# V tiles by head, filled by one transfer and two halo copies, with q and k loaded further ahead in a fused attention and two-layer feed-forward kernel

## The reference, cut to what matters

```python
def _attn_ref(q, k, v):                     # block 32, window 16
    k_sum = k.reshape(B, H, nb, block, D).max(axis=3)
    v_sum = v.reshape(B, H, nb, block, D).mean(axis=3)
    scores_l = scale * q @ k.T, kept where |i - j| < window
    scores_s = scale * q @ k_sum.T + log(block)
    a = softmax(concat(scores_l, scores_s))
    return a @ concat(v, v_sum)

x = attention, heads side by side           # (1536, 512)
h = x @ w_in;  solu = h * softmax(h);  x = layernorm(solu) * g_ln @ w_out
h = x @ w2_in; out = elu(h) @ w2_out
```

## Time and profile before

| | us |
|---|---|
| median of 3 runs | 538.21 |
| lowest and highest | 536.62, 539.1 |
| the profiled execution | 538.56 |
| its span, first to last instruction | 536.8 |

### The profile page before, as it was taken

One profiled execution on the slowest core, in us unless ns is written; L12 is line 12 of the kernel. 1 busy time (PEld: TensorE's weight loads), 2 busy tenths in 40 slices (PEclk: granted clock), 3 DMA queues, 4 the chain that ended last, 5 costly groups with the idle time before them and its releaser, 6 DMA issues.

```text
span 536.8 us, 8565 instructions
## 1 busy us (share of the span) xinstructions
PE 502.4 (94%) x3312; PEld 420.5 (78%) x3312; DVE 235.5 (44%) x625; ACT 212.6 (40%) x433; POOL 112.3 (21%) x100
## 2 busy tenths in 40 slices
PE   3698879897999999999999999999999999999997
PEld 2476657675779889899988888888888888888885
DVE  2445644652684255455256454423233333333231
ACT  2346634751574346345455443324121223222222
POOL 2263838440012002002445353200000000000000
PEclk9999965999899999999999999999999999999999
DMA  9579596934000000017000000002000002000002
GB/s 176 115 137 229 130 216 147 227 118 206 0 0 2 1 0 1 1 45 269 1 1 0 1 0 2 0 1 78 1 0 0 1 0 78 0 0 0 0 0 78
DMA packets 46402, 30.35 MB, mean 57 GB/s; under 512 B 40096, under 2 KB 40096, under 8 KB 45472
## 3 DMA queue, kind: packets, MB, share of 16 engines
q1 hardware_dynamic: 46368, 29.89, 21.6%
HBM read 25.17 MB, written 3.15 MB: 53 GB/s over the span
## 4 chain that ended last, share of the span: by engine, by line
PE 80%; DMA 5%; SPq 4%; POOL 4%; DVE 3%; ACT 2%; issue 2%; DVEq 0%; POOLq 0%
PE bank L854 12%; PE bank L856 12%; PE bank L855 12%; PE bank L1056 8%; PE bank L1057 8%; PE bank L1055 8%; PE bank L1011 4%; PE bank L1013 4%; PE bank L1012 4%; DMA vblocks<-in_v 3%; PE bank L931 2%; POOL vblocks L406 2%; SPq L311 2%; PE bank L997 2%; PE bank L898 1%
## 5 line engine op out<-in xcount | busy, mean ns | idle before, releaser
L615 ACT ACTIVATE ex<-bank 128x512 f32<-128x512 f32 x48 | 28.7, 598 | 127.9 <-PE bank L856 127.9
L856 PE MATMUL bank<-yt_lo,w2in_hi 128*128 (+1 forms) x192 | 74.7, 389 | 0.0
L855 PE MATMUL bank<-yt_hi,w2in_lo 128*128 (+1 forms) x192 | 74.7, 389 | 0.0
L1055 PE MATMUL bank<-w2out_hi,g_hi 128*128 128x512 f32 x192 | 74.7, 389 | 0.0
L1056 PE MATMUL bank<-w2out_lo,g_hi 128*128 128x512 f32 x192 | 74.7, 389 | 0.0
L854 PE MATMUL bank<-yt_hi,w2in_hi 128*128 (+1 forms) x192 | 74.7, 389 | 0.0
L1057 PE MATMUL bank<-w2out_hi,g_lo 128*128 128x512 f32 x192 | 74.7, 389 | 0.0
L832 DVE TENSOR_SCALAR ex<-ex 128x512 f32<-128x512 f32 x48 | 21.6, 450 | 116.5 <-ACT ex L615 116.5
L837 DVE TENSOR_TENSOR g_lo<-gf,g_hi 128x512 fp32r<-128x512 f32 x48 | 46.5, 969 | 35.9 <-ACT g_hi L623 35.9
L623 ACT ACTIVATE g_hi<-gf 128x512 fp32r<-128x512 f32 x48 | 30.3, 632 | 49.0 <-DVE gf L834 49.0
L498 ACT ACTIVATE se<-se,nm 128x120 f32<-128x120 f32 x96 | 32.5, 387 | 36.4 <-DVE nm L683 36.4
(11 more groups left out here) (103 smaller groups left out, 845.1 us busy)
## 6 DMA issues: line engine op xcount, KB each, us to landing
w2in_raw<-in_w_in SPq DMA_DIRECT2D x1, 4096.0 KB, 12.3
w2out_raw<-in_w_out SPq DMA_DIRECT2D x4, 1024.0 KB, 9.4
kraw<-in_k SPq DMA_DIRECT2D x16, 192.0 KB, 5.3
qraw<-in_q SPq DMA_DIRECT2D x16, 192.0 KB, 4.0
vblocks<-in_v SPq DMA_DIRECT2D x4, 768.0 KB, 8.8
out<-osb SPq DMA_DIRECT2D x12, 256.0 KB, 2.1
vw<-in_v SPq DMA_DIRECT2D x16, 176.0 KB, 6.1
win_raw<-in_w_in SPq DMA_DIRECT2D x4, 512.0 KB, 6.1
```

Of the source, the lines that this page charges most:

```text
L855: pe.matmul(acc, al, bh, start=False, stop=False)
L856: last = pe.matmul(acc, ah, bl, start=False, stop=(i == n - 1))
L1055: pe.matmul(dst, g_hi[:, j % GS, cols], w2out_hi[:, j, :], start=(j == 0), stop=False)
```

## The change

Three things change together.

- vw has its heads outside its windows. One transfer brings both heads' 768 rows to partitions 16 to 79 (64 partitions, 12 windows of each head). Two copies inside SBUF fill the halos: partitions 64 to 79 of each window go to partitions 0 to 15 of the next, and partitions 16 to 31 go to partitions 80 to 95 of the one before. The zeros, the means copy and the matmuls follow the layout.
- Raw k and q have four slots each instead of two.
- SP's list is another one. vblocks(0) stands ahead of q(0), fill_halo(0) ahead of move_means(0), and v(1), vblocks(1), k(2), q(2) are issued ahead of the loop. In round n it is: fill_halo(n + 1), v(n + 2), move_means(n/2 + 1) and vblocks(n/2 + 2) if n is even, k(n + 3), q(n + 3), then w_in or w_out.

```diff
-        (kt, qraw), a1 = place(W2IN, ("kt", [P, 2, HALO + S + HALO], F32), ("qraw", [P, 2, T, P], F32))
+        RAWS = 4
+        (kt, kraw, qraw), a1 = place(
+            W2IN, ("kt", [P, 2, HALO + S + HALO], F32), ("kraw", [P, RAWS, T, P], F32),
+            ("qraw", [P, RAWS, T, P], F32))
...
-            LN, ("kraw", [P, 2, T, P], F32), ("vw", [P, VS, SUBS, 2, D1], F32),
+            LN, ("vw", [P, VS, 2, SUBS, D1], F32),
...
             def load_k(n):
-                if n >= 2:
-                    sp.wait_ge(kv_in_psum, n - 1)
+                if n >= RAWS:
+                    sp.wait_ge(kv_in_psum, n - RAWS + 1)
...
                 else:
                     sp.wait_ge(attn_done, T * (n - VS + 1))
-                for h in range(2):
-                    body = vf[2 * n + h, HALO:HALO + (SUBS - 1) * SUB, :].rearrange("(j i) d -> i j d", i=SUB)
-                    sp.dma_start(vw[2 * HALO:LOCAL, s, 0:SUBS - 1, h, 0:D], body).then_inc(v_loaded[s], 16)
-                sp.dma_start(vw[HALO:2 * HALO, s, 0, :, 0:D],
-                             vf[2 * n:2 * n + 2, 0:HALO, :].rearrange("h i d -> i h d")).then_inc(v_loaded[s], 16)
-                sp.dma_start(vw[2 * HALO:2 * HALO + REST, s, SUBS - 1, :, 0:D],
-                             vf[2 * n:2 * n + 2, S - REST:S, :].rearrange("h i d -> i h d")).then_inc(v_loaded[s], 16)
+                sp.dma_start(vw[HALO:HALO + SUB, s, :, :, 0:D].rearrange("i h j d -> i (h j) d"),
+                             vf[2 * n:2 * n + 2].rearrange("h (j i) d -> i (h j) d", i=SUB)).then_inc(v_loaded[s], 16)
 
             def fill_halo(n):
 
                 s = n % VS
-                sp.wait_ge(v_loaded[s], 16 * V_DMAS * (n // VS + 1))
-                sp.dma_start(vw[0:2 * HALO, s, 1:SUBS, :, :],
-                             vw[SUB:LOCAL, s, 0:SUBS - 1, :, :]).then_inc(halo_filled[s], 16)
+                if n == 0:
+                    sp.wait_ge(zeros_ready, 2)
+                sp.wait_ge(v_loaded[s], 16 * (n // VS + 1))
+                sp.dma_start(vw[0:HALO, s, :, 1:SUBS, :], vw[SUB:SUB + HALO, s, :, 0:SUBS - 1, :]).then_inc(halo_filled[s], 16)
+                sp.dma_start(vw[SUB + HALO:LOCAL, s, :, 0:SUBS - 1, :], vw[HALO:2 * HALO, s, :, 1:SUBS, :]).then_inc(halo_filled[s], 16)
...
             load_k(0)
+            load_vblocks(0)
             load_q(0)
-            load_vblocks(0)
             load_v(0)
             load_k(1)
+            fill_halo(0)
             move_means(0)
-            fill_halo(0)
             load_q(1)
+            load_v(1)
+            load_vblocks(1)
+            load_k(2)
+            load_q(2)
             for n in range(PAIRS):
+                if n + 1 < PAIRS:
+                    fill_halo(n + 1)
+                if n + 2 < PAIRS:
+                    load_v(n + 2)
                 if n % 2 == 0 and n // 2 + 1 < MEANS:
-                    load_vblocks(n // 2 + 1)
-                if n + 1 < PAIRS:
-                    load_v(n + 1)
-                if n + 2 < PAIRS:
-                    load_k(n + 2)
-                    load_q(n + 2)
+                    move_means(n // 2 + 1)
+                if n % 2 == 0 and n // 2 + 2 < MEANS:
+                    load_vblocks(n // 2 + 2)
+                if n + 3 < PAIRS:
+                    load_k(n + 3)
+                    load_q(n + 3)
...
-                if n + 1 < PAIRS:
-                    fill_halo(n + 1)
-                if n % 2 == 0 and n // 2 + 1 < MEANS:
-                    move_means(n // 2 + 1)
...
-            dve.memset(vw[:, :, 0, :, 0:D], 0.0)
-            dve.memset(vw[:, :, SUBS - 1, :, 0:D], 0.0).then_inc(zeros_ready, 1)
+            dve.memset(vw[0:HALO, :, :, 0, 0:D], 0.0)
+            dve.memset(vw[SUB:P, :, :, SUBS - 1, 0:D], 0.0).then_inc(zeros_ready, 1)
```

More of the change, by code:

```diff
@@ L126, in fused_layers_kernel @@
         (vblocks,), _ = place(3 * KD * F1 * 4, ("vblocks", [NB * HPM, 2, BLOCK * D], F32))
-        (kraw, vw, qt, se, pt, vmean, ks, mt, mask, bands, xn), a2 = place(
-            LN, ("kraw", [P, 2, T, P], F32), ("vw", [P, VS, SUBS, 2, D1], F32),
+        (vw, qt, se, pt, vmean, ks, mt, mask, bands, xn), a2 = place(
+            LN, ("vw", [P, VS, 2, SUBS, D1], F32),
             ("qt", [P, 2, S], F32), ("se", [P, RING, 2, KEYS], F32),
@@ L164, in fused_layers_kernel @@
         pool_step = sem("pool_step")
-        k_loaded = [sem("k_loaded0"), sem("k_loaded1")]
-        q_loaded = [sem("q_loaded0"), sem("q_loaded1")]
+        k_loaded = [sem(f"k_loaded{i}") for i in range(RAWS)]
+        q_loaded = [sem(f"q_loaded{i}") for i in range(RAWS)]
         v_loaded = [sem("v_loaded0"), sem("v_loaded1"), sem("v_loaded2")]
@@ L247, in fused_layers_kernel @@
         block = ctx.enter_context(nc.Block())
-        V_DMAS = 4
-        REST = S - HALO - (SUBS - 1) * SUB
+        HALO_DMAS = 2
         T_LAG, PV_LAG, X_LAG = 2, 3, 6
@@ L266, in load_k @@
             def load_k(n):
-                if n >= 2:
-                    sp.wait_ge(kv_in_psum, n - 1)
+                if n >= RAWS:
+                    sp.wait_ge(kv_in_psum, n - RAWS + 1)
                 for h in range(2):
-                    sp.dma_start(kraw[:, n % 2, :, h * D:(h + 1) * D],
-                                 pair_of_heads(kf, n)[:, :, h, :]).then_inc(k_loaded[n % 2], 16)
+                    sp.dma_start(kraw[:, n % RAWS, :, h * D:(h + 1) * D],
+                                 pair_of_heads(kf, n)[:, :, h, :]).then_inc(k_loaded[n % RAWS], 16)
             def load_q(n):
-                if n >= 2:
-                    sp.wait_ge(q_in_psum, n - 1)
+                if n >= RAWS:
+                    sp.wait_ge(q_in_psum, n - RAWS + 1)
                 for h in range(2):
-                    sp.dma_start(qraw[:, n % 2, :, h * D:(h + 1) * D],
-                                 pair_of_heads(qf, n)[:, :, h, :]).then_inc(q_loaded[n % 2], 16)
+                    sp.dma_start(qraw[:, n % RAWS, :, h * D:(h + 1) * D],
+                                 pair_of_heads(qf, n)[:, :, h, :]).then_inc(q_loaded[n % RAWS], 16)
             def load_v(n):
@@ L318, in load_vblocks, with load_win, load_wout @@
                              ).then_inc(vblocks_loaded[c % 2], 16)
+            def load_win(i):
+                sp.dma_start(win_raw[:, i, :], w_in[i * P:(i + 1) * P, :]).then_inc(win_loaded[i], 16)
+            def load_wout(i):
+                sp.dma_start(wout_raw[:, 2 * i:2 * i + 2, :],
+                             w_out[2 * i * P:(2 * i + 2) * P, :].rearrange("(k p) n -> p k n", p=P)
+                             ).then_inc(wout_loaded[i], 16)
             load_k(0)
+            load_vblocks(0)
             load_q(0)
-            load_vblocks(0)
             load_v(0)
             load_k(1)
+            fill_halo(0)
             move_means(0)
-            fill_halo(0)
             load_q(1)
+            load_v(1)
+            load_vblocks(1)
+            load_k(2)
+            load_q(2)
             for n in range(PAIRS):
+                if n + 1 < PAIRS:
+                    fill_halo(n + 1)
+                if n + 2 < PAIRS:
+                    load_v(n + 2)
                 if n % 2 == 0 and n // 2 + 1 < MEANS:
-                    load_vblocks(n // 2 + 1)
-                if n + 1 < PAIRS:
-                    load_v(n + 1)
-                if n + 2 < PAIRS:
-                    load_k(n + 2)
-                    load_q(n + 2)
+                    move_means(n // 2 + 1)
[4 more added lines that the diff above has]
+                    load_q(n + 3)
                 if n == 0:
@@ L340, in _ @@
                 if n < KD:
-                    i = n
-                    sp.dma_start(win_raw[:, i, :], w_in[i * P:(i + 1) * P, :]).then_inc(win_loaded[i], 16)
+                    load_win(n)
                 if n >= 4:
[L344 to L347, removed]
-                if n + 1 < PAIRS:
-                    fill_halo(n + 1)
-                if n % 2 == 0 and n // 2 + 1 < MEANS:
-                    move_means(n // 2 + 1)
+                    load_wout(n - 4)
             sp.wait_ge(scores_in_psum, UNITS)
@@ L435, in spread_means @@
                 pool.tensor_copy(vw[LOCAL:KEYS, s, :, :, 0:D],
-                                 mt[LOCAL:KEYS, c, None, i:i + 2, :].broadcast_to([NB, SUBS, 2, D])
+                                 mt[LOCAL:KEYS, c, i:i + 2, None, :].broadcast_to([NB, 2, SUBS, D])
                                  ).then_inc(means_spread, 1)
@@ L859, in prep_k @@
             def prep_k(n):
-                s = n % 2
-                pe.wait_ge(k_loaded[s], 32 * (n // 2 + 1))
+                s = n % RAWS
+                pe.wait_ge(k_loaded[s], 32 * (n // RAWS + 1))
                 if n == 0:
@@ L879, in prep_q @@
                     pe.wait_ge(xlo_ready, 2 * n - 3)
-                pe.wait_ge(q_loaded[s], 32 * (n // 2 + 1))
+                pe.wait_ge(q_loaded[s], 32 * (n // RAWS + 1))
                 for t in range(T):
@@ L922, in attend @@
                 if t == 0:
```

(4 more changed lines are left out.)

## The result

| | before | after |
|---|---|---|
| median us (4 runs each) | 538.65 | 560.7 |
| lowest and highest | 536.62, 540.97 | 559.76, 562.33 |
| profiled execution, its span | 538.56, 536.8 | 559.76, 558.0 |

The ratio is 1.041 (95% interval 1.036 to 1.046). The forecast was 559 us, range 546 to 567.

The account below looks back on a forecast made before the run. Attention was taken as bound by a loop through SP, GpSimd and DMA, not by TensorE. 538.6 us + 14.9 for the longer loop + 5 for the clock = 558.5, said as 559 us, range 546 to 567.

Parts of the forecast that it names:

- The loop: SP, DMA and GpSimd, means to means: two pairs would take 34.1 us, against 26.2 before the change.
- The start: Before the loop: vblocks(0) issued 1.2 us earlier, first attend at about 19.9 instead of 21.40, means(1) ready at about 33.3.
- TensorE, which I had 2 us ahead: TensorE at prep_q(1): some 2 us earlier than before the change, bounds 0 and 2.8.
- Attend of pair 2: TensorE would arrive at about 48 us and stall some 5 us, until spread_means(2) at 54.
- After means(3): End of attention: moves 3.2, loads 6.6 + 1.7, split 3.5, spread 1.5 us, then attend of pair 6.
- The sum for pair 6: Attend of pair 6 on TensorE at 118.0 us against 103.12 before: +14.9 us.
- The clock: TensorE from pair 6 on: a stall of at least 3 us may halve its clock, +5 us, bounds 0 and +9.
- The halo copies at nothing: Two halo copies instead of one: no added time, bounds -0.7 to +0.7 us each, hidden behind SP's wait for means.
- SP spared about 1 us a pair: SP's V issues: two fewer at 0.7 us each, at most 1.4 us a pair, about 1 in the sum.
- rival 2: V's transfer to 64 unevenly spread rows takes twice as long: +4 us, 563; sign: V over 3.5 us; chance 0.05.
- Rival 3: Attention's loads do keep ahead, so stalls go and low clock shrinks: 16 us faster, 522.6; chance 0.08.
- Rival 5: Every stall drops the clock and full rings hold SP before win(i), 2 us more per loop: +28, 566.5; chance 0.12.

## Why the prediction held, term by term

**The loop: right, and the cause.** Predicted 34.1 us; 36.2 and 34.4 measured. From means(1): moves 3.2, transfers 21.9 in the first loop and 20.0 in the second (predicted 20.0), splits, spread and adds 11.1 (10.9). The new order with the old tile reproduces it, and the two edits to its sides bear it out: with the weights ahead of the moves, less stands between means and odd split, and the loop is 30 us (28 expected); with the spread ahead of the split, which the loop holds either way, it stays at 35.

**The start: wrong.** I had means(1) ready 1.3 us earlier than before, at 33.3; they were moved at 35.77. Two things made the 2.5 us. First, the prediction had the moves of means(0) begin near 14 and left out that fill_halo(0) now stands ahead of them. The means were ready at 13.3 (DVE's timeline), but SP waited for v(0), which landed at 13.6 (the chain), and issued two halo copies; the moves began at 15.04. So vblocks(1) was issued at 20.19, where the sum implies about 19.3. Here are the rows of DVE, of the chain and of SP:

```profile
13.07 0.19 DVE L724 TENSOR_SCALAR vmean<-vmean 96x64 f32<-96x64 f32 x1
...
3.48 10.13 DMA vw<-in_v
20.19 9.54 DMA vblocks<-in_v
...
13.70 0.66 SPq L298 DMA_DIRECT2D vw<-vw  x1
```

Second, vblocks(1) took 9.54 us, not 7.99 as before, and landed at 29.73; I had 27.3, with v(1) alone as new in front of it. From the issue of v(1) at 19.46 to that landing the queue moved 205 GB/s, 2.1 MB, and v(1), vblocks(1) and the rest of q(1) are at most 1.6: part of k(2) and q(2), issued behind, moved with them. The first half of k(2), issued at 21.34, landed 0.2 us before vblocks(1).

TensorE, which I had 2 us ahead, was 1.5 us ahead at prep_q(1) (22.60 against 24.10), and level with before when it reached attend of pair 2 (50.3 against 50.0). In the first pair, q(0) behind vblocks(0) cost it 5.03 us of waiting, which the later wait for V's means hid. Attend of pair 2 waited 7.37 us, where I had some 5.

**After means(3):** 17.0 us to attend of pair 6, predicted 16.5.

**The sum for pair 6:** 123.35, predicted 118.0; so +20.2 and not +14.9. Of the 5.3 us, 2.5 are the start, 2.3 the two loops, 0.5 the rest.

**The clock: mis-sized the other way.** I took +5 us between bounds of 0 and 9. TensorE did wait 4.8 us before pair 6 and did go on at the low clock, but the clock had not fallen there: it fell at 115.0, behind the 2.70 us wait for k(7) and 8 us before pair 6 went on. The 13.7 us at the low level ran through the stall, and only 5.3 us of them were left for pair 6:

```profile
110.00:115.00 5.00, 2.30 (x54) 1.89 (x50) 0.94 (x5) 2.22 (x7) 0.00 (x0) 1.00 0.91 207
115.00:123.30 8.30, 3.54 (x43) 2.24 (x35) 3.56 (x14) 2.61 (x7) 4.83 (x3) 0.50 0.89 170
123.40:128.60 5.20, 5.20 (x60) 4.18 (x62) 1.00 (x9) 1.83 (x5) 4.74 (x3) 0.50 0.80 237
128.80:131.00 2.20, 2.20 (x53) 1.63 (x47) 2.00 (x9) 1.43 (x5) 2.12 (x2) 1.00 0.05 11
```

From attend of pair 6 to the first dense matmul 14.91 us passed (123.35 to 138.26), against 13.56 before: +1.35. Two errors of about 4 and 5 us so cancelled, which is luck, and 559 is nearer to 560.7 than its terms deserve: 538.6 + 20.2 + 1.35 = 560.2, and the profiled execution took 559.76.

**The halo copies at nothing, SP spared about 1 us a pair: not seen.** In the tile alone V's issues are shorter, but those of k and q behind them are longer. From the issue of V to that of the weights SP took 4.8, 10.3, 4.8, 10.0 and 5.7 us before, and 5.7, 11.0, 4.7, 10.6 and 5.1 with the tile alone. V itself, from issue to landing, was 1.8 us slower in the first of three, 0.4 in the second, and 0.4 faster in the third. Alone the tile costs 0.5% (rival 2 had 4 us for it); inside the changed kernel it shows in no difference (1.041 and 1.043). The sign that the prediction gave for rival 2, a V of over 3.5 us, tells nothing: the old tile's four took 4.1 us or more as well.

**The other rivals.** Rival 3, that the loads keep ahead, did not come. Its price, 522.6 us, would need no stall at all; the best order found here gave 529.4. Rival 5's held issues were there (SP took 4.03 us for q(3)) but inside the loop's transfer time, so nothing was added; that full rings held them no row shows.

**What is right in the idea.** With q and k loaded further ahead, the old tile, and both lists put in another order, the kernel is 1.8% faster than before. Step by step, the weights, then k and q, then the halo came ahead of SP's wait for means, with GpSimd's spread and adds moved too, and until the last step the stall went on to the next thing in the list. How much of the 1.8% is the loads ahead, and how much the order, is not shown: no run has that order with two slots, or the old list with four.

## What to carry to other kernels

When a list with waits is reordered, write down for each wait everything behind it on that queue and who needs it, and follow the circle back to the wait: a loop through two engines (here SP waits for GpSimd's sums, GpSimd waits for weights that SP issues behind them) sets the pace, and four buffers instead of two did not help. When a stall is removed, look at what is next behind the same wait before pricing the gain; in several of the runs the stall just went on to the next transfer. Keep transfers with an early consumer and no wait of their own ahead of every wait.

## What the runs showed of the hardware

- Six transposes cost 0.85 or 1.54 us, and how long the low clock lasts varied: 70.8 to 91.3 us before the change, around the 3.33 us stall, and 115.0 to 128.7 in the changed kernel, from behind a 2.70 us wait and through a 4.82 us one. TensorE was busy for 19.5 of the first 20.5 us and for 8.9 of the second 13.7. No run here explains the difference.
- The same 384 KB in 256-byte rows took 4.9, 4.1 and 4.8 us to partitions 32 to 95, and 5.9, 4.7 and 5.3 us to 16 to 79, in kernels that are otherwise nearly alike, behind the moves of means(1), (2) and (3).
- A vblocks transfer of 768 KB took 5.8 us where the queue was idle before it and k and q followed (38.96 and 75.15 in the changed kernel), 8.0 us behind q(1) and ahead of v(1) and k(2) (20.57 before the change), and 9.5 us with q(1) and v(1) ahead of it and k(2) and q(2) behind (20.19 in the changed kernel). Completion is not in the order of issue either: in the last case half of k, issued 1.2 us later, landed 0.2 us earlier.
